# Two attention steps per round on 64x64 state corners, x kept in SBUF, and feed-forward weights fetched block by block

## Time and profile before

| | |
|---|---|
| Runs | 1132.38, 1132.20, 1131.48 us, median 1132.2 |
| Profiled execution, span | 1128.4 us (first to last instruction) |
| PE busy | 1089.5 us (97%) |
| DVE, ACT, POOL busy | 450.2 (40%), 282.7 (25%), 119.5 us (11%) |
| Granted TensorE clock, mean | 0.992 |
| Moved by DMA | 102.80 MB |

### The profile page before, as it was taken

How to read it: one execution, slowest core, us unless ns; L and a number is a source line. 1 busy time by engine, 2 the same in 40 slices (tenths; PEclk the granted TensorE clock), 3 DMA queues, 4 the chain that set the end, 5 groups by cost and what they waited for, 6 DMA issues and landing times.

```text
span 1128.4 us, 18320 instructions
## 1 busy us (share of the span) xinstructions
PE 1089.5 (97%) x6313; PEld 978.0 (87%) x6314; DVE 450.2 (40%) x857; ACT 282.7 (25%) x489; POOL 119.5 (11%) x105
## 2 busy tenths in 40 slices
PE   7888999999999999999999999998999999999997
PEld 6777899999998999998999999996788888888885
DVE  5888521222221322221232222339464544454542
ACT  2333221212211112111211112114043433343421
POOL 3444100000000000000000000004111111112111
PEclk9999999999999999999999999998899999999999
DMA  9999300100101001001001000014535343335310
GB/s 334 356 368 358 131 1 1 57 1 1 57 1 55 3 1 56 1 1 58 1 1 56 1 1 29 1 32 165 186 133 182 126 167 130 109 112 191 117 33 33
DMA packets 43350, 102.80 MB, mean 91 GB/s; under 512 B 4062, under 2 KB 20702, under 8 KB 43297
## 3 DMA queue, kind: packets, MB, share of 16 engines
q1 hardware_dynamic: 38816, 88.15, 22.3%
q0 software_dynamic: 4480, 13.90, 3.6%
HBM read 83.15 MB, written 19.66 MB: 91 GB/s over the span
## 4 chain that ended last, share of the span: by engine, by line
PE 89%; DMA 5%; DVE 3%; issue 1%; POOL 1%; SPq 1%; ACT 0%; POOLq 0%; DVEq 0%; ACTq 0%
PE bank L713 36%; PE bank L727 18%; PE bank L1085 13%; PE bank L1064 12%; DMA rows<-in_steps 5%; PE bank L1071 2%; PE bank L539 1%; PE bank L367 1%; PE bank L382 1%; PE bank L423 1%; PE bank L375 1%; PE bank L533 1%; POOL k_dec L284 1%; PE bank L358 0%; PE bank L783 0%
## 5 line engine op out<-in xcount | busy, mean ns | idle before, releaser
L713 PE MATMUL bank<-x_hi,w_hi 128*128 128x384 f32 x768 | 258.4, 336 | 5.2 <-issue 3.4
L713 PE MATMUL bank<-x_hi,w_lo 128*128 128x384 f32 x768 | 257.8, 336 | 0.0
L713 PE MATMUL bank<-x_lo,w_hi 128*128 128x384 f32 x768 | 257.2, 335 | 0.0
L665 DVE TENSOR_TENSOR g_sb<-bank,b_sb 128x384 f32<-128x384 f32 x96 | 53.5, 557 | 407.8 <-PE bank L713 407.8
L713 PEld LDWEIGHTS bank<-x_hi,w_hi 128*128 128x128 f32 x768 | 144.2, 188 | 9.9 <-issue 6.2
L713 PEld LDWEIGHTS bank<-x_lo,w_hi 128*128 128x128 f32 x768 | 144.2, 188 | 3.6
L713 PEld LDWEIGHTS bank<-x_hi,w_lo 128*128 128x128 f32 x768 | 144.1, 188 | 0.0
L497 ACT COPY b_sb<-bank 128x384 f32<-128x384 f32 x96 | 46.0, 479 | 283.4 <-PE bank L713 283.4
L727 PE MATMUL bank<-w_hi,g_hi 128*128 128x512 f32 x288 | 116.0, 403 | 0.0
L727 PE MATMUL bank<-w_hi,g_lo 128*128 128x512 f32 x288 | 113.6, 394 | 0.0
L727 PE MATMUL bank<-w_lo,g_hi 128*128 128x512 f32 x288 | 113.3, 393 | 0.0
(11 more groups left out here) (154 smaller groups left out, 1309.7 us busy)
## 6 DMA issues: line engine op xcount, KB each, us to landing
raw<-in_w SPq DMA_DIRECT2D x64, 512.0 KB, 5.9
rows<-in_steps SPq DMA_DIRECT2D x48, 512.0 KB, 7.6
w_raw<-in_weights SPq DMA_DIRECT2D x12, 768.0 KB, 8.5
xT_dram<-attn_sb SPq DMA_DIRECT2D x24, 256.0 KB, 6.0
x_raw<-xT_dram SPq DMA_DIRECT2D x8, 768.0 KB, 5.7
x_dram<-y_sb SPq DMA_DIRECT2D x8, 768.0 KB, 4.3
mask_t<-in_consts SPq DMA_DIRECT2D x1, 512.0 KB, 6.3
xg<-x_dram,idx_gather POOLq DMA_INDIRECT x28, 3.6
```

Of the source, the lines that this page charges most:

```text
L665: nc.vector.tensor_tensor(g_sb[:, f % 2], bank[2 * (f % 2)][:, 0:GT], b_sb[:, f % 2], ALU.mult).then_inc(g_done, 1)
L713: ins = nc.tensor.matmul(bank[to][:, 0:GT], w[:, j, cols], x[s][:, k, :], start=(k == 0 and m == 0), stop=(k == KD - 1 and m == 2))
```

## The change

**Attention in rounds.** Two steps make a round (`ROUND` = 2, 3 rounds a batch). `rows` has six slots, one for each step of a batch, and a round of the next batch is loaded when `within` of the same round of this batch is done. PE's order in the loop is: scores of the next round, cross of this, state products of the next, within of this. `probs` has three buffers; scores go to banks 0 to 3.

**64x64 corners.** `states` keeps only the 64x64 diagonal corners, four buffers deep. The state products are 8 matmuls of 64 columns a step instead of 4 of 128 (bank 6; none for the last step of a batch). Cross is 8 matmuls a step of 64 rows and 64 columns of the array (none for the first step of a batch). Output of the two steps of a round is in banks 4 and 5, and ACT copies it in four pieces of 64 partitions into `x_all`. The decay and the addition are one instruction for each pair on DVE (`scalar_tensor_tensor`, 4 a step). The memsets of the state and the decay on POOL are gone, and `q_dec` moves from DVE to POOL, behind `k_dec` in its program.

**x in SBUF.** `x_all` holds all of x. Groups 0 and 1 are split from it (`split_ready_hi`, `split_ready_lo`) between the last rounds. Groups 2 to 7 are stored to `xT_dram` by one DMA each and loaded again as before.

**Weights in group one.** No weights are fetched in attention but `load_wab(0)` and `load_wo(0)`, which SP issues after the last load of rows. The layout is by pairs of blocks (`wab`, 1 MB each, 1 KB per row) and triples (`wo`, 768 KB). ACT and DVE split them a block at a time: blocks 0 and 1 at the end of attention, block f + 2 inside block f of group 0. `up` waits for its block's `wab_lo` and `down` for its `wo_lo`.

The core of the diff:

```diff
+        for c in range(1, CH):
+            load_step(0, c)
...
         with sp.Fori(0, B - 1) as b:
-            batch(b, False)
-        batch(B - 1, True)
-        for s in range(2):
-            sp.wait_ge(xT_out[s], 16 * (STEPS // 2) + 16)
+            for j in range(RB):
+                sp.wait_ge(attn_done, round_no(b, j) + 1 + CREDIT)
+                for i in range(ROUND):
+                    load_step(b + 1, ROUND * j + i)
+        load_wab(sp, 0)
+        load_wo(sp, 0)
+        sp.wait_ge(attn_read, (B - 1) * RB + CREDIT)
+        for g in range(READY, (B - 1) * CH * P // GT):
+            store_x(sp, g)
+
+    def sp_weights(sp):
+
+        sp.wait_ge(attn_done, ROUNDS + CREDIT)
+        load_wab(sp, 1)
+        sp.wait_ge(attn_read, ROUNDS + CREDIT)
+        for g in range((B - 1) * CH * P // GT, GROUPS):
+            store_x(sp, g)
+        sp.wait_ge(xT_out, 16 * (GROUPS - READY))
+        sp.wait_ge(x_lo_done, READY * KD)
+        load_wab(sp, 2)
+        load_wo(sp, 1)
+        load_wab(sp, 3)
+        load_wo(sp, 2)
+        load_wab(sp, 4)
+        load_wo(sp, 3)
+        load_wab(sp, 5)
...
+        def decays(b, j):
+            first = isinstance(b, int) and b == 0 and j == 0
+            for i in kv_steps(j):
+                c = ROUND * j + i
+                pool.wait_ge(kv_in[c], (b + 1) * 16)
+                if i == 0 and not first:
+                    pool.wait_ge(kv_done, round_no(b, j))
+                nc.gpsimd.tensor_tensor(k_dec[:, i].rearrange("p (h d) -> p h d", h=H),
+                                        rows[:, c, 2].rearrange("p (h d) -> p h d", h=H),
                                         kdec, ALU.mult).then_inc(k_dec_done, 1)
...
+            for i in range(ROUND):
+                c = ROUND * j + i
+                pool.wait_ge(rows_in[c], (b + 1) * 16)
+                if first and i == 0:
+                    pool.wait_ge(qdec_in, 16)
+                if i == 0 and not first:
+                    pool.wait_ge(cross_done, round_no(b, j))
+                nc.gpsimd.tensor_tensor(q_dec[:, i], rows[:, c, 0], qdec_t, ALU.mult).then_inc(q_dec_done, 1)
...
+        def evict(b, j):
+            act.wait_ge(attn_done, round_no(b, j) + 1 + CREDIT)
+            for o in range(2):
+                for e in range(2):
+                    frm, to = slice((o ^ e) * D, (o ^ e) * D + D), slice(o * D, (o + 1) * D)
+                    ins = nc.scalar.copy(x_all[to, e::2, bass.ds((b * CH + ROUND * j) * P, ROUND * P)].rearrange("p a (i t) -> p i a t", i=ROUND),
+                                         bank[4 + o][frm, :].rearrange("p (i a t) -> p i a t", i=ROUND, a=PAIRS // 2))
+            ins.then_inc(attn_read, 1)
+
+        with act.Fori(0, B - 1) as b:
+            for j in range(RB):
+                evict(b, j)
+        evict(B - 1, 0)
+        split_ready_hi(act, 0)
+        evict(B - 1, 1)
+        split_ready_hi(act, 1)
+        split_w_hi(act, 0)
+        evict(B - 1, 2)
+        split_w_hi(act, 1)
...
+        def new_states(b, j):
+            dve.wait_ge(kv_done, round_no(b, j) + 1)
+            for i in kv_steps(j):
+                c = ROUND * j + i
+                kv = bank[6][:, i * PAIRS * D:(i + 1) * PAIRS * D].rearrange("p (a e) -> p a e", a=PAIRS)
+                if c == 0:
+                    nc.vector.tensor_copy(states[:, 1], kv).then_inc(state_new, 1)
+                    continue
+                dve.wait_ge(state_new, b * (CH - 1) + c)
+                for p in range(PAIRS):
+                    ins = nc.vector.scalar_tensor_tensor(states[:, (c + 1) % 4, p], states[:, c % 4, p], kdec_t[:, H + p:H + p + 1],
+                                                         kv[:, p], ALU.mult, ALU.add)
+                ins.then_inc(state_new, 1)
...
+        def out_at(i, p, o):
+            c0 = (o ^ (p % 2)) * D
+            return bank[4 + o][c0:c0 + D, (i * (PAIRS // 2) + p // 2) * P:(i * (PAIRS // 2) + p // 2 + 1) * P]
+
+        def cross(b, j):
+            pe.wait_ge(attn_read, round_no(b, j) + CREDIT)
...
+                for p in range(PAIRS):
+                    for o in range(2):
+                        half_p, corner = slice(o * D, (o + 1) * D), (o, p % 2)
+                        ins = nc.tensor.matmul(out_at(i, p, o), states[half_p, c % 4, p, :], q_dec[half_p, i, p * P:(p + 1) * P],
+                                               start=corner not in opened, stop=False, skip_group_check=True)
...
+        scores(0, 0)
+        kv(0, 0)
+        with pe.Fori(0, B - 1) as b:
+            for j in range(RB):
+                scores(*following(b, j))
+                cross(b, j)
+                kv(*following(b, j))
+                within(b, j)
...
@@ -498,8 +637,10 @@
                 act.wait_ge(g_done, n + 1 + 2)
                 act.wait_ge(down_done, n - 1 + 2)
                 nc.scalar.copy(g_hi[:, f % 2], g_sb[:, f % 2]).then_inc(g_hi_done, 1)
-                if f == 3 and not last:
+                if f == 3 and not first and not last:
                     split_x_hi(act, g + 1, 1 - s)
+                if first and f + 2 < KF:
+                    split_w_hi(act, f + 2)
...
@@ -701,16 +843,15 @@
 
             n = g * KF + f
             pe.wait_ge(g_done, n - 1 + 2)
-            if f == 0 and isinstance(g, int) and g == 0:
-                pe.wait_ge(w_lo_done, STEPS)
-            cols = slice(f * P, (f + 1) * P)
+            if isinstance(g, int) and g == 0:
+                pe.wait_ge(w_lo_done, 2 * f + 1)
```

More of the change, by code:

```diff
@@ L21 @@
 STEPS = B * CH
-SLOTS = 3
+ROUND = 2
+RB = CH // ROUND
+ROUNDS = STEPS // ROUND
 KD = DM // P
 KF = DF // P
-PIECES = 3 * KD
+HALVES = KF // 2
+THIRDS = KF // 3
 GT = 384
@@ L124, in build, with wo_place, wab, wo @@
     common = at[0]
-    w_hi = place("w_hi", (P, PIECES, DF), F32R)
+    wab_hi_at = at[0]
+    wab_hi = place("wab_hi", (P, HALVES, 2 * KD, 2 * P), F32R)
+    wo_hi = place("wo_hi", (P, THIRDS, 3 * DM), F32R)
     w_lo_at = at[0]
-    w_lo = place("w_lo", (P, PIECES, DF), F32R)
-    w_raw = place("w_raw", (P, PIECES, DF), F32, where=w_lo_at)
-    after_w = at[0]
[L132 to L143, removed]
+    wab_lo = place("wab_lo", (P, HALVES, 2 * KD, 2 * P), F32R)
+    wo_lo_at = at[0]
+    wo_lo = place("wo_lo", (P, THIRDS, 3 * DM), F32R)
+    wab_raw = place("wab_raw", (P, HALVES, 2 * KD, 2 * P), F32, where=w_lo_at)
+    wo_raw = place("wo_raw", (P, THIRDS, 3 * DM), F32, where=wo_lo_at)
+    after_w = at[0]
+    half_bytes, early = 2 * KD * 2 * P * 4, 2
+    rows = place("rows", (P, CH, 4, DM), where=wab_hi_at + early * half_bytes)
+    x_all = place("x_all", (P, KD, NT), where=w_lo_at + early * half_bytes)
+    assert CH * 4 * DM * 4 <= (HALVES - early) * half_bytes + (THIRDS - 1) * 3 * DM * 4
+    assert KD * NT == CH * 4 * DM
+    def wo_place(u):
+        return (u + THIRDS - 1) % THIRDS
+    def wab(w, f, j):
+        return w[:, f // 2, j, (f % 2) * P:(f % 2 + 1) * P]
+    def wo(w, f):
+        return w[:, wo_place(f // 3), (f % 3) * DM:(f % 3 + 1) * DM]
     at[0] = after_w
@@ L150, in build @@
     x_hi, x_lo = (x0_hi, x1_hi), (x0_lo, x1_lo)
+    kdec_t = place("kdec_t", (P, H + PAIRS))
+    small_at = at[0]
+    qdec_t = place("qdec_t", (P, PAIRS * P))
+    mask_t = place("mask_t", (P, H, P))
+    q_dec = place("q_dec", (P, ROUND, PAIRS * P))
+    k_dec = place("k_dec", (P, ROUND, DM))
+    states = place("states", (P, 4, PAIRS, D))
+    probs = (place("probs0", (P, ROUND, H, P)),
+             place("probs1", (P, ROUND, H, P), where=wab_hi_at + half_bytes),
+             place("probs2", (P, ROUND, H, P), where=w_lo_at + half_bytes))
+    small_end = at[0]
+    at[0] = small_at
     b_sb = place("b_sb", (P, 2, GT))
@@ L157, in build @@
     yT_sb = place("yT_sb", (P, KD, P))
+    x_raw_at = max(at[0], yT_sb_at + 3 * DM * 4)
+    x_raw = place("x_raw", (P, KD, GT), where=x_raw_at)
     at[0] = x_raw_at
@@ L291, in act_attention @@
-    def act_attention(act):
[L292 to L301, removed]
@@ L465, in group @@
         def group(g, s, first, last):
-            if not last:
+            if first:
+                sp_weights(sp)
+            elif not last:
                 sp.wait_ge(x_lo_done, KD * (g + 1))
@@ L711, in up @@
                     j = which * KD + k
-                    for m, (w, x) in enumerate(((w_hi, x_hi), (w_hi, x_lo), (w_lo, x_hi))):
-                        ins = nc.tensor.matmul(bank[to][:, 0:GT], w[:, j, cols], x[s][:, k, :],
+                    for m, (w, x) in enumerate(((wab_hi, x_hi), (wab_hi, x_lo), (wab_lo, x_hi))):
+                        ins = nc.tensor.matmul(bank[to][:, 0:GT], wab(w, f, j), x[s][:, k, :],
                                                start=(k == 0 and m == 0), stop=(k == KD - 1 and m == 2))
```

250 lines of the change are left out of this document (137 added, 113 removed).

## The result

The changed kernel takes 1106.05 us (median of 4 runs, 1104.45 to 1108.22), the kernel before 1132.2 us: 0.9769 of it, 95% interval 0.975 to 0.9788, 26 us faster. The profiled execution took 1108.22 us and has a span of 1106.4 us. It is the slowest of the four, and the four follow the mean granted clock: 0.985, 0.990, 0.992 and 0.990 for 1108.22, 1106.43, 1104.45 and 1105.66 us. A mean of 0.985 in 1106 us is 33 us at half clock, 0.992 is 18 us.

The account below looks back on a forecast made before the run. Transfers were taken to bound attention: 42 MB at 356 GB/s, 118 us. The first feed-forward matmul 30.2 us earlier, with 0 for group one and later work, gave 1132.2 - 30.2 = 1102.0 us; range 1096 to 1117.

Parts of the forecast that it names:

- the right case: Whole kernel: the forecast outcome, 1096 to 1108 us, given a chance of 0.58.
- A round, T = 6.7 us: Two steps on PE: 2.35 scores and eviction wait, 1.2 cross, 1.0 state products, 1.8 within, 0.4 hand-overs; bounds 6.1 to 8.4.
- The start: Attention's prologue: rounds 0 and 1 wait for landing keys and values; round 1 ends at 27.1 us, nine rounds count from 27.3.
- Nine rounds: Attention after round 1: nine rounds of T, 60.3 us, ending at 87.6 us; DMA bounds the first three rounds only.
- The tail, 6.8 us: End of attention: eviction, x_hi, w_hi, w_lo and hand-overs take 6.8 us, so the first feed-forward matmul starts at 94.4 us.
- Group one: First feed-forward group with its weights arriving: 0 us lost, bounds 0 and 4; wo 1 has 1 us to spare.
- t0: Attention: the end of the eleventh `within`, forecast at 87.6 us.
- The same work, 0: Groups two to eight and the experts: same work as before, 0 us change.
- The bound before: Attention of the kernel before: 42 MB of transfers at 356 GB/s, 118 us, with PE and DVE limits close behind.
- tiles that start in strict order: Rival, attention on PE: cross runs two corners at once, within takes 1.5 times; T 8.1, 1116 us; chance 0.17.
- Late weights: Rival, group one: wo 1 lands at t0 + 30, 5 us lost, 1107 us; chance 0.12.
- stay at 1.2 GHz in small corners: Rival, attention: small corners keep TensorE at 1.2 GHz; T 11.8, 1153 us, slower than before; chance 0.04.

Follow-up runs that it names:

- after_plain: The changed kernel with PE's three loads of a tile's expert in the expert stage made bounded loads plus a register move; base of the variants: 1106.79 us.
- after_two_copies: Base with banks 4 and 5 emptied by one 128x512 copy each instead of two of 64x512, rows of w_a and w_b reordered to match: 1101.18 us.
- after_three_edits: Base with two copies for the eviction, the activation table loaded before the loop, and q, kT and k of the next batch fetched earlier: 1092.43 us.
- both experiments on corners: Base with cross's pairs ordered 0, 2, 1, 3: 1106.93 us; base with all cross matmuls on two corners first, then the other two: 1112.41 us.

## Why the prediction was right

The forecast was 1102.0 us, measured 1106.05, inside 1096 to 1117: the right case, and 4 us too far. In `after_plain`, where the clock held through attention, the first `up` is 2.5 us later than forecast and the address of g_hi costs 1.6 us, which together are the 4 us. Point by point, by its own steps:

- **A round, T = 6.7 us.** Undisturbed rounds take 6.68 and 6.34 us. The sum is right by luck, because its errors cancel: cross cost 1.04 us for two steps and 0.59 for one, 0.9 on average and not 1.2 (the floor, four at once, not 0.6 a step); state products 0.8 and not 1.0; the four hand-overs 0 and not 0.4. Against that the eviction was mis-sized. It was put at 2.1 us, from three copies in 1.57; here four take 2.35, each 0.59 behind the last, and cross waits 0.76 to 0.86 beyond scores, not 0.4. A copy of 64 partitions costs what one of 128 does (0.58 and 0.59 us). One sum is off: all ceilings together give 8.8 us, not 8.4; the range did not rest on it. The 0.17 us for a change of shape stand in the earlier trace rows only before scores, though the sum takes them three times; in the changed kernel the weight loads idle for them before state products and before scores (1.5 us in nine times each, from 28 to 90 us).
- **The start.** The second round ended at 28.1 us, not 27.3. The first of the three table loads (at 20.7 us) and a wait of 1.21 us for ACT lie before it.
- **Nine rounds.** They took 62.7 us (28.1 to 90.8), not 60.3. The step that failed is "Two rounds are fetched ahead of use". A round's loads are issued when its `within` ends, and the next batch's scores for it come two iterations later in the loop, so one whole iteration lies between: 6.3 us, against a landing of 6.2 us in the median. Waits for `rows` came at 36, 43, 79 and 86 us. The table load was left out altogether; it takes 1.3 us in each of three rounds, two of them among these nine, and taking all three away gave 3.3 us. So was the clock: it fell behind a wait of 2.05 us (cross, at 66.1) and behind one of 2.55 (at 93.3), and made 1.92 us of `within` into 3.18 and 3.56. The same two waits stand in `after_plain`, and there the clock held, so they alone don't decide it.
- **The tail, 6.8 us.** 7.1 us, with another cause: ACT and DVE were done in time, and the last `within` at the low clock set the start. In `after_plain`, where the clock held, w_lo released the first `up`, as forecast, after 6.6 us.
- **Group one.** Block 1's w_lo, called tight, was a gap of 0.50 us. `wo` 1, given 1 us to spare, was just in time in the changed kernel (0.31 us late in `after_plain`), and 1.23 and 0.93 us late in `after_two_copies` and `after_three_edits`. In `after_plain` ACT began to split it at t0 + 25.1 us, where 24 was forecast, and that used the slack up. The named place was right and its slack too large.
- **Nothing behind it.** "The same work, 0" missed 1.6 us: g_hi and its neighbours moved by 64 bytes.
- **The bound before.** That the transfers bound attention was true and less than I made of it: taking the weights away from the old order gave 6.3 us, and with the old traffic the new loop still gives 12.4, with the stores in longer rows.

Of the rivals, tiles that start in strict order (1116 us) is ruled out by the changed kernel, where two steps of cross take 1.04 us and not 1.8, and by both experiments on corners. The rule of the Trainium skill's page "TensorE: Matmul & The Clock Gate", Part 3, that matmuls start in program order doesn't describe the times here. Late weights cost nothing in the changed kernel and 0.31 us in `after_plain`, against 5 in the rival: `wo` 1 came at t0 + 25, not 30. PE didn't stay at 1.2 GHz in small corners: the granted clock is 0.98 from 20 to 90 us, with cross at 64x64.

## What to carry to other kernels

When one bound is lifted, price each edge of the new cycle by the instruction that releases it, and count the iterations between the issue of a load and its first wait in the program text, not in the number of buffers. Edges that lie at the same place hide one another: taken away singly, two gave 5.9 and 3.3 us and the third nothing, together 11.7. An eviction is paid by its columns, so an output placed in halves of partitions doubles it, unless the order of the rows can be mended in the weights' layout.

## What was not expected of the hardware

- The table of ACT is loaded again in every pass of the loop (three passes, three loads of 1.28 us); one tiny copy ahead of the loop ends that.
- A `down` matmul of 512 columns became slower by an address: 0.2 us in a group of 108 such matmuls, 2 ns each, when its stationary operand and the tiles behind it stood 64 bytes off a multiple of 512 from x.
- PE fills a free 64x64 corner from further back in its program: an order with 8 instructions for two corners in a row costs 0.05 us in 1.1, one with 16 costs 0.5.
- DMA engines that are busy all the time move 356 GB/s in one loop and 400 in another. A packet of 512 bytes took 27 ns, one of 1 KB 46 ns, one of 4 KB 159 ns in the median.
